# Seven block products for eight in the w_in product of a recurrence and feed-forward kernel

## The reference, cut to what matters

```python
sig = 1.0 / (1.0 + np.exp(-f_logit))
f = lower_bound + (1.0 - lower_bound) * sig
for t in range(S):
    h = f[:, t] * h + (1.0 - f[:, t]) * x[:, t]
    y[:, t] = h
h = y @ w_in                                  # (12160, 256) x (256, 2048)
g = np.where(h >= 1, h, np.where(h <= -1, 0.0, (h + 1) ** 2 / 4.0))
out = g @ w_out                               # (12160, 2048) x (2048, 256)
```

## Time and profile before

| | |
|---|---|
| median of 3 runs | 1079.61 us (1079.31 to 1081.16) |
| span of the profiled execution | 1077.3 us; clock 1.000 |
| around the span (median less span) | 2.3 us |
| PE busy | 1068.0 us (99%), 4,632 matmuls with 24 of the warm-up |
| DVE, ACT, POOL busy | 804.1 us, 451.2 us, 0.2 us |
| DMA | 41.76 MB, 39 GB/s |

### The profile page before, as it was taken

One profiled execution on the slowest core, in us unless ns is written; L12 is line 12 of the kernel. 1 busy time (PEld: TensorE's weight loads), 2 busy tenths in 40 slices (PEclk: granted clock), 3 DMA queues, 4 the chain that ended last, 5 costly groups with the idle time before them and its releaser, 6 DMA issues.

```text
span 1077.3 us, 11996 instructions
## 1 busy us (share of the span) xinstructions
PE 1068.0 (99%) x4632; PEld 868.4 (81%) x4632; DVE 804.1 (75%) x741; ACT 451.2 (42%) x476; POOL 0.2 (0%) x4
## 2 busy tenths in 40 slices
PE   7999999999999999999999999999999999999998
PEld 4788888888888888888888888888888888888887
DVE  7976867778777677786776877868677787776764
ACT  6443444434444344443443434434444344443432
POOL 0000000000000000000000000000000000000000
PEclk9999999999999999999999999999999999999999
DMA  7110101101011010110101101101011010100000
GB/s 272 39 39 20 58 0 58 57 1 58 7 51 58 0 58 19 39 58 0 58 21 37 58 0 58 45 13 58 0 58 58 0 58 14 44 19 1 20 19 19
DMA packets 20010, 41.76 MB, mean 39 GB/s; under 512 B 2336, under 2 KB 15136, under 8 KB 20000
## 3 DMA queue, kind: packets, MB, share of 16 engines
q1 hardware_dynamic: 20000, 41.63, 11.3%
HBM read 29.16 MB, written 12.45 MB: 39 GB/s over the span
## 4 chain that ended last, share of the span: by engine, by line
PE 96%; DVE 3%; DMA 0%; ACT 0%; issue 0%; SPq 0%; DVEq 0%
PE acc L369 16%; PE acc L368 16%; PE h L367 16%; PE acc L367 16%; PE h L369 16%; PE h L368 16%; DVE g L304 1%; DVE g L299 1%; DVE y L287 0%; DMA gate<-f_logit_chunks 0%; DVE g_lo L309 0%; DVE w_out_lo L268 0%; DVE w_in_lo L264 0%; DVE drive L280 0%; DVE gate L273 0%
## 5 line engine op out<-in xcount | busy, mean ns | idle before, releaser
L209 ACT ACTIVATE g<-h 128x1016 f32<-128x1016 f32 (+1 forms) x192 | 195.4, 1018 | 603.8 <-PE h L369 603.8
L299 DVE SCALAR_TENSOR_TENSOR g<-g 128x1016 f32<-128x1016 f32 (+1 forms) x192 | 232.7, 1212 | 259.9 <-ACT g L209 259.9
L367 PE MATMUL h<-y_hi,w_in_lo 128*128 128x508 f32 (+1 forms) x768 | 302.3, 394 | 4.9 <-DVE g L304 2.9
L369 PE MATMUL acc<-g_hi,w_out_hi 128*128 128x508 f32 (+1 forms) x768 | 301.2, 392 | 0.0
L368 PE MATMUL acc<-g_lo,w_out_hi 128*128 128x508 f32 (+1 forms) x768 | 301.1, 392 | 0.0
L369 PE MATMUL h<-y_hi,w_in_hi 128*128 128x508 f32 (+1 forms) x768 | 300.3, 391 | 0.0
L367 PE MATMUL acc<-g_hi,w_out_lo 128*128 128x508 f32 (+1 forms) x768 | 300.3, 391 | 0.0
L368 PE MATMUL h<-y_lo,w_in_hi 128*128 128x508 f32 (+1 forms) x768 | 299.6, 390 | 0.0
L309 DVE TENSOR_TENSOR g_lo<-g,g_hi 128x1016 fp32r<-128x1016 f32 (+1 forms) x192 | 231.7, 1207 | 1.1 <-ACT g_hi L214 1.1
L304 DVE TENSOR_TENSOR g<-g,h 128x1016 f32<-128x1016 f32 (+1 forms) x192 | 230.8, 1202 | 0.0
L214 ACT CAST g_hi<-g 128x1016 fp32r<-128x1016 f32 (+1 forms) x192 | 197.9, 1031 | 7.2 <-DVE g L304 7.2
(11 more groups left out here) (16 smaller groups left out, 82.2 us busy)
## 6 DMA issues: line engine op xcount, KB each, us to landing
gate<-f_logit_chunks SPq DMA_DIRECT2D x48, 254.0 KB, 2.8
drive<-x_chunks SPq DMA_DIRECT2D x48, 254.0 KB, 4.1
out_chunks<-result SPq DMA_DIRECT2D x22, 508.0 KB, 2.7
w_in_f<-w_in_pairs SPq DMA_DIRECT2D x8, 256.0 KB, 5.6
w_out_f<-w_out_pairs SPq DMA_DIRECT2D x8, 256.0 KB, 7.3
out_chunks<-result SPq DMA_DIRECT2D x1, 492.0 KB, 3.8
out_chunks<-result SPq DMA_DIRECT2D x2, 246.0 KB, 2.0
lb<-lower_bound_tiles SPq DMA_DIRECT2D x1, 1.0 KB, 2.4
```

The costliest lines, as they stand in the source:

```text
L209: nc.scalar.activation(g[:, slot, :, 0:width], h[:, h_slot, :, 0:width], ACT.Relu, bias=0.5, scale=0.5).then_inc(t_ready, 1)
L299: nc.vector.scalar_tensor_tensor(out=t, in0=t, scalar=1.0, in1=t, op0=ALU.min, op1=ALU.mult).then_inc(square_ready, 1)
L367: nc.tensor.matmul(dst, w_lo, v_hi, start=start, stop=False)
L369: return nc.tensor.matmul(dst, w_hi, v_hi, start=False, stop=stop)
```

## The change

The w_in product is now done on blocks of two by two by two: two feature tiles, two column blocks, and even and odd tokens of one batch, 1,024 tokens at a time (960 in the first and last of 12 spans). That is eight block products; by the Strassen-Winograd scheme seven are enough. Seven combinations of blocks of w_in stand in `w_in_hi` and `w_in_lo` (A11, A12, A22, sums S1 to S4), and seven terms of y (E0, E1: even tokens of the two feature tiles, O1: odd tokens of the second, T1 to T4: differences) in `terms_hi` and `terms_lo`.

The sums of products are formed in PSUM where they can be: the bank `chain` takes A11 E0, then S2 T2 on top, then S3 T3, then A22 T4, and ACT copies the bank out after each of the first three (`copy_p1`, `copy_u2`, `copy_u3` into `part`). `side` holds A12 E1, and `cross` holds S1 T1, later with S4 O1 on top. DVE adds a copy and a bank for three of the four results (`add_h11`, `add_h22`, `add_h12`, into `h`); the fourth, H21, is read in `chain`. The activation is now one of 512 elements for each result: relu and square on ACT (the square moved there), minimum and maximum in one DVE instruction, the high part on ACT, the low part on DVE. A window (`window`, one per pair of column blocks and span) has the seven products and between them the eight w_out products of the window before.

POOL gets the gates (`forget`), the sums of w_in's blocks, w_in's low parts and the differences of y (`t1` to `t4`). `result` is single and filled at every second column, with one store for a span. The diff, cut to its core; in the DVE window the branches of the first span are left out:

```diff
@@ constants and names @@
-ROUNDS = 12
-CHUNK = 508
+SPANS = 12
+FULL, SHORT = 512, 480
-WARM_UP = 24
+WARM_UP = 36
-H_SLOTS = 2
-G_SLOTS = 4
-AHEAD = 3
+A11, S3, A12, A22, S1, S2, S4 = range(TERMS)
+E0, E1, O1, T1, T2, T3, T4 = range(TERMS)
+COLUMNS = {H11: 0, H22: 1, H21: 1, H12: 0}
+TOKEN = {H11: 0, H22: 1, H21: 0, H12: 1}
...
+        chain = psum("chain", [P, 2, BANK])
+        side = psum("side", [P, BANK])
+        cross = psum("cross", [P, BANK])
+        acc = psum("acc", [P, 2, KT, BANK])
@@ gpsimd @@
+            def sums(j):
+                pool.wait_ge(w_in_loaded[j], 16)
+                term = w_in_f[:, j]
+                nc.gpsimd.tensor_tensor(term[:, S1], term[:, S3], term[:, A22], ALU.add).then_inc(sums_ready, 1)
+                pool.wait_ge(sums_ready, 4 * j + 1)
+                nc.gpsimd.tensor_tensor(term[:, S3], term[:, A11], term[:, S3], ALU.subtract).then_inc(sums_ready, 1)
+                nc.gpsimd.tensor_tensor(term[:, S2], term[:, S1], term[:, A11], ALU.subtract).then_inc(sums_ready, 1)
+                pool.wait_ge(sums_ready, 4 * j + 3)
+                nc.gpsimd.tensor_tensor(term[:, S4], term[:, A12], term[:, S2], ALU.subtract).then_inc(sums_ready, 1)
...
+            forget_half(0, 0)
+            forget_half(0, 1)
+            sums(0)
+            forget_half(1, 0)
+            forget_half(1, 1)
+            t1(0)
+            weights_low(0)
+            t3(0)
+            for k in range(KT):
+                save(0, k)
+            for j in range(1, PAIRS):
+                sums(j)
+                weights_low(j)
+            for q in range(1, SPANS):
+                for k in range(KT):
+                    forget(k, slice(0, 2 * width(q)), 4 * q + 2 * k + 2, 2)
+                save(q, 0)
+                t1(q)
+                save(q, 1)
+                t3(q)
+                t2(q)
+                t4(q)
@@ scalar @@
...
+            def window(q, j, cols, before, after, after_slot, first=False):
+                w = PAIRS * q + j
+                slot = j % 2
+                copy_p1(w, slot, cols)
+                if before:
+                    g_high(w - 1, H21, before)
+                    relu_added(w - 1, H12, before)
+                relu_added(w, H11, cols)
+                if before:
+                    square(w - 1, H12, before)
+                square(w, H11, cols)
+                copy_u2(w, slot, cols)
+                if before:
+                    g_high(w - 1, H12, before)
+                g_high(w, H11, cols)
+                if first:
+                    out_high(j)
+                    if j < 2:
+                        in_high(2 * j + 2)
+                    if j in (2, 3):
+                        sigmoid(q + 1, j - 2, after)
+                    if j == 6:
+                        act.wait_ge(w_in_lo_ready, PAIRS)
+                        even_high(q + 1, after_slot, after)
+                    if j == 7:
+                        t_pair_high(q + 1, after_slot, 0, after)
+                elif after:
+                    if j in (1, 2):
+                        sigmoid(q + 1, j - 1, after)
+                    if j == 5:
+                        even_high(q + 1, after_slot, after)
+                    if j == 6:
+                        t_pair_high(q + 1, after_slot, 0, after)
+                copy_u3(w, slot, cols)
+                if first:
+                    if j < 2:
+                        in_high(2 * j + 3)
+                    if j in (2, 3):
+                        in_high(j + 4)
+                    if j == 6:
+                        odd_high(q + 1, after_slot, after)
+                    if j == 7:
+                        t_pair_high(q + 1, after_slot, 1, after)
+                else:
+                    if j == 0:
+                        evacuate(q - 1, 0, before)
+                    if after and j == 5:
+                        odd_high(q + 1, after_slot, after)
+                    if after and j == 6:
+                        t_pair_high(q + 1, after_slot, 1, after)
+                relu_added(w, H22, cols)
+                square(w, H22, cols)
+                relu_chain(w, slot, cols)
+                square(w, H21, cols)
+                g_high(w, H22, cols)
+                if j == 0 and not first:
+                    evacuate(q - 1, 1, before)
...
+            for k in range(KT):
+                for n in range(2):
+                    sigmoid_half(k, n)
+            in_high(0)
+            even_high(0, 0, width(0), slice(0, 1))
+            even_high(0, 0, width(0), slice(1, 2))
+            odd_high(0, 0, width(0))
+            for n in range(4):
+                t_high(0, 0, n, width(0))
+            in_high(1)
@@ vector @@
+            def add(t, cols, one, bank):
+                nc.vector.tensor_tensor(h[:, ADDED[t], 0:cols], part[:, one, 0:cols], bank[:, 0:cols],
+                                        ALU.add).then_inc(h_added[t], 1)
...
+            def window(q, j, cols, before, after, b, after_slot, first=False):
+                w = PAIRS * q + j
+                if before:
+                    add_h12(w - 1, before)
+                    g_low(w - 1, H22, before)
+                add_h11(w, cols)
+                if before:
+                    g_low(w - 1, H21, before)
+                    activated(w - 1, H12, h[:, ADDED[H12], 0:before], before)
+                activated(w, H11, h[:, ADDED[H11], 0:cols], cols)
+                if first and j == 7:
+                    odd_low(q + 1, after_slot, after)
+                if before:
+                    g_low(w - 1, H12, before)
+                g_low(w, H11, cols)
...
+                elif after:
+                    if j == 2:
+                        drive(q + 1, 0, after)
+                    if j == 3:
+                        scan(q + 1, b, 0, 1, after)
+                    if j == 4:
+                        scan(q + 1, b, 1, 0, after)
+                    if j == 6:
+                        odd_low(q + 1, after_slot, after)
+                    if j == 7:
+                        t_pair_low(q + 1, after_slot, 1, after)
+                add_h22(w, cols)
...
+                elif after:
+                    if j == 2:
+                        scan(q + 1, b, 0, 0, after)
+                    if j == 3:
+                        drive(q + 1, 1, after)
+                    if j == 4:
+                        scan(q + 1, b, 1, 1, after)
+                    if j == 5:
+                        even_low(q + 1, after_slot, after)
+                    if j == 6:
+                        t_pair_low(q + 1, after_slot, 0, after)
+                activated(w, H22, h[:, ADDED[H22], 0:cols], cols)
+                activated(w, H21, chain[:, j % 2, 0:cols], cols)
...
+            for k in range(KT):
+                for n in range(2):
+                    drive_half(k, n)
+                    scan(0, 0, k, n, cols)
+                if k == 0:
+                    even_low(0, 0, cols, slice(0, 1))
+            dve.wait_ge(t_ready[0], 1)
+            dve.wait_ge(y_ready, 4)
+            nc.vector.tensor_tensor(t_term(1, cols), odd(1, cols), t_term(0, cols), ALU.subtract).then_inc(t_ready[1], 1)
+            even_low(0, 0, cols, slice(1, 2))
+            dve.wait_ge(t_ready[1], 1)
+            nc.vector.tensor_tensor(t_term(3, cols), even(1, cols), t_term(1, cols), ALU.subtract).then_inc(t_ready[3], 1)
+            odd_low(0, 0, cols)
+            for n in range(4):
+                t_low(0, 0, n, cols)
@@ tensor @@
+            def product(dst, j, weight, s, term, cols, start):
+                return three_passes(dst[:, 0:cols], w_in_hi[:, j, weight], w_in_lo[:, j, weight],
+                                    terms_hi[s][:, term, 0:cols], terms_lo[s][:, term, 0:cols], start, True,
+                                    more=not start)
...
+            def window(q, j, s, cols, before, first=False):
+                w = PAIRS * q + j
+                jp = (j - 1) % PAIRS
+                qp = q if j else q - 1
+                line = chain[:, j % 2]
+                def operand(term):
+                    if j == 0:
+                        pe.wait_ge(terms_ready, TERMS * q + term + 1)
+                if first:
+                    pe.wait_ge(w_in_lo_ready, j + 1)
+                operand(E0)
+                if not first or j > 1:
+                    pe.wait_ge(g_ready[H21], w - 1)
+                product(line, j, A11, s, E0, cols, True).then_inc(p1_ready, 1)
+                operand(E1)
+                if before:
+                    pe.wait_ge(h_added[H11], w)
+                product(side, j, A12, s, E1, cols, True).then_inc(p2_ready, 1)
+                if before:
+                    if first:
+                        pe.wait_ge(w_out_lo_ready, jp + 1)
+                    elif j == 0:
+                        pe.wait_ge(w_out_lo_ready, PAIRS)
+                    second_h11(w - 1, qp, jp, before)
+                operand(T2)
+                pe.wait_ge(p1_copied, w + 1)
```

(79 more changed lines are left out.)

599 lines of the change are left out of this document (338 added, 261 removed).

## The result

| | before | changed |
|---|---|---|
| time, median | 1079.84 us (1079.31 to 1081.16, 4 runs) | 1098.07 us (1096.54 to 1100.12, 4 runs) |
| ratio, 95% interval | | 1.0161 (1.0149 to 1.0173) |
| span of the profiled execution | 1077.3 us | 1094.7 us |

The forecast was 1037 us, with a range of 1022 to 1074. The kernel became 1.6% slower, with 288 matmuls fewer in its products (276 with those of the warm-up).

What follows compares the result with a forecast made beforehand. PE was taken as the bound, by count and width of its matmuls: start 34.3, PE's work 989.1, rest of span 0 1, end 1.9 + 5.3, waits 3 make 1034.6 us; plus 2.3 around the span, 1037 us, range 1022 to 1074.

Steps and rivals of the forecast that it cites:

- PE's work: Matmul time on PE over the run: 3,600 matmuls of 512 columns and 720 of 480, 989.1 us, down 65.8 us.
- No wait is late: PE's waits in the windows: copies and additions come in time, the second copy with 0.1 to 0.9 us of room; 3 us allowed.
- side product done at 1.6, addition to 2.3: Path to a window's second copy, in us: DVE's addition follows the side product, then relu to 3.0; copy needed at 5.54.
- Rival C: ACT becomes the bound because its instructions don't overlap, pitch 0.66 us; 67 us more, 1101 us; chance 0.10.
- Rival B: POOL's instructions in each span hold DVE back and a part reaches PE; 1053 us likelier, 1070 at most; chance 0.25.
- POOL's price: POOL's arithmetic taken at twice DVE's time, with DVE's price as low end and four times that as high end.
- The start: Until window 2 is done at 58.6 us: 34.3 us are not PE work; third product at 21.9 us.
- The ring of ACT and POOL: At the start, ACT's casts of blocks 3 and 5 wait for POOL's low parts and sums, 2.2 + 2.3 us a block.
- Rest of span 0: Windows of span 0 after the start, with ACT at 9.8 of 9.9 us a window: 1 us lost.
- The time around the span: Run time outside the profiled span, added at the end: 2.3 us.
- the last span: Span 11 and the end, with late last-window paths, evacuation and final store: 7.2 us.

Runs made afterwards that it cites:

- e7: The kernel before with its four operand tiles of 508 columns laid in rows of 512, width of the work still 508: 1069.63 us, ratio 0.9893.
- e8: The kernel before with tiles of 512 columns (a last one of 448) in place of 508: 1066.80 us, ratio 0.9868.
- e5: The changed kernel with ACT's square of H12 moved ahead of the relu of H11: 1080.65 us, ratio to before 0.9999.
- e6: The changed kernel with three steps of ACT and one of DVE in another order, no instruction more or less: 1060.30 us, ratio to before 0.9809.
- e3: The changed kernel with POOL's gates and differences from span 1 on cut to 8 columns, waits and signals kept: 1087.77 us, ratio to before 1.0069.
- e4: The changed kernel with w_in's low parts on DVE, POOL's first gates ahead of its sums, first tile's even tokens rounded ahead of w_in's block: 1084.65 us.
- e1: The changed kernel with the loops of ACT, DVE and PE over pairs of spans written out: 1081.40 us, ratio to before 1.0011.

## Why the prediction was wrong

- **PE's work**: right in kind, 17 us too high. I extended a line through 492 and 508 columns to 512. e7 shows that the row length moves the pitch too; 2.2 ns between e8 and the changed kernel stay open. This error made the kernel faster than forecast and hides 17 us of the others.
- **"No wait is late" failed**, and it is the step that cost the forecast. I had "side product done at 1.6, addition to 2.3": DVE was taken as free when the operand came. In the rows DVE's addition of H11 starts 2.9 us into its window (511.51, window from 508.60), because ahead of it in DVE's order stand the maximum of H21, the addition of H12 and a low part, and the first of these waits for the tail of ACT's last window. Relu to 3.0 was 4.3, the copy at 4.0 was 5.2, its end 5.8 where 5.4 is needed. I had walked the path within one window, and never closed it over the window's border. PE's waits were 46.7 us over 80 windows, 0.58 us each on average, where I had put 3 us over the run. e5 and e6, which only move instructions, take 17.4 and 37.8 us off, so it is shown that the waits come from the order. What they test is the place of the squares in the path and not the late addition: in e6 the addition of H11 still starts 2.1 to 3.1 us into its window (2.5 to 3.9 in the changed kernel; both without the windows at back edges), and PE hardly waits, since no square stands between relu and copy. That the late addition used up the room is read from the rows, not tested alone.
- **Rival C** came nearest in time (1101) for a wrong reason: ACT's casts and squares still follow at 0.52 to 0.54 us, and e6 needs not one instruction less.
- **Rival B** and contention: 10.3 us by e3, where 16 to 33 were given. POOL's gates were also shorter than forecast: the median of L212 is 1.21 us, for 2.2. DVE's scan at 507.11 took 1.64 us for 1.28 beside a gate on POOL. The Trainium skill (SBUF — State Buffer, Who interferes with whom) has the pair exclude each other for the whole instruction; the overlap was 0.57 us (the gate ran from 505.79 to 507.68) and the scan 0.36 longer, so here the rows show a part of that. The gate, which began behind DVE's drive at 505.38, was longer as well, 1.89 us.
- **POOL's price** of twice DVE's held for the low parts of w_in: the 896-element low part took 2.08 to 2.48 us (2.2 forecast).
- **The start**: 34.3 us were 41.7, the third product at 27.5 for 21.9. The ring of ACT and POOL was foreseen; two things were not. The lower clock: steps of 0.40 us at 480 columns until 36.6 us, for 0.217 behind that. And ACT's first copy, at 26.78, stands in ACT's queue behind the cast of w_in's second block, which waits for POOL's sums (e4 kept this, so its third product gained only 1.3 us):
```profile
25.94 0.94 ACT L298 CAST w_in_hi<-w_in_f 128x896 fp32r<-128x896 f32 x1 [2.21 <-POOL w_in_f L226]
```
- **Rest of span 0**: 11.4 us for 1. I counted ACT's instructions per window, and not that POOL's gates of span 1 stand behind all of its sums and low parts. In e4, with the low parts off POOL, the fourth window is 6.2 us shorter, of 13.4 us over the whole start.
- **Back edges**: not in the sum at all. ACT had the same loop before, but idled for 596 us behind PE; I did not ask what that idle time covered. 16.7 us by e1.
- The time around the span (1.8 us for 2.3) and the last span (8.1 for 7.2) were close.

Of the 60 us between the forecast span and the profiled one, the waits in the windows are 44, the back edges 15, the start with the rest of span 0 18, the end 1, less 17 for the pitch.

## What to carry to other kernels

When instructions on in-order engines depend on each other in both directions, find the closed path that returns to its first instruction one period later, add up its steps with what stands ahead of each in its engine's order, and compare that sum with the period; here it was 9.52 us of 10.20, while ACT was busy for 80% and DVE for 77%, shares that show nothing of it. Then order instructions by what lies on that path: here that was worth 38 us without one instruction less. And before an idle engine is loaded, list what its idle time has been hiding, loop back edges first.

## What was not expected of the hardware

- A back edge of ACT's loop left it idle for 4.3 to 4.5 us, and made the window 4.9 us longer on PE: 3.8 us without work, and 1.6 us at the lower clock behind it, less about 0.5 for a wait that such a window has otherwise. In five other runs with the loop ACT was idle for 4.3 to 4.9 us.
- After a wait that is late the step to the next matmul is mostly 0.34 us (0.30 to 0.34), for 0.227.
- Rows of 512 instead of 508 for the same 508 columns took 11 us (1%) off the kernel before.
